# Sixteen products of 64 columns in place of three of 512 ahead of TensorE's attention loop

## The chip, the cores and the metric

The kernel runs on one core of a Trainium2 chip. The metric is the device time of one execution in microseconds (us), given as a median of several executions.

## The reference

Local attention feeds a mixture of experts, which feeds a second block with a SoLU layer. Cut to its core:

```python
def reference(**kwargs):
    # attention: batch 4, heads 8, 768 rows, head width 64; chunks of 32 rows,
    # each sees 16 rows to its left, 8 to its right and 8 memory rows
    for c in range(nc):
        k_full = np.concatenate([mem_k, k[:, :, l_start:r_end]], axis=2)
        v_full = np.concatenate([mem_v, v[:, :, l_start:r_end]], axis=2)
        scores = scale * np.matmul(q_c, k_full.transpose(0, 1, 3, 2))
        a = np.exp(scores - np.max(scores, axis=-1, keepdims=True))
        a = a / (np.sum(a, axis=-1, keepdims=True) + 1e-09)
        out[:, :, c_start:c_end] = np.matmul(a, v_full)
    x = out.transpose(0, 2, 1, 3).reshape(3072, 512)
    # experts: each token goes to one of 8, at most 384 tokens each, best logits first
    logits = x @ w_gate
    for e in range(8):
        h = np.maximum(x[assigned == e] @ w1[e], 0.0)
        y[assigned == e] = h @ w2[e]
    h = y @ w_in                      # 512 -> 1024
    solu = h * softmax(h)
    ln = (solu - mean) / sqrt(var + 1e-06) * g_ln
    return ln @ w_out
```

## The kernel before, in words

The program is written engine by engine: each engine has its own block of code, and the order in it is the order of execution. Semaphores alone join the engines. There is no scheduler.

The attention works on NT = 24 tiles of 128 token rows. For each tile, SyncE loads one packed tile of q and k (`unit`, 768 KB, four buffers) and one of v (`vr`, 520 KB, four buffers). TensorE's code for it is the function `step` (called at L510 in a loop `pe.Fori(0, NT // DEEP)` of six passes, four steps in each pass). A step holds, in this order, pieces of different tiles, as a pipeline written out by hand:

- `x_T` (L478): four transposes of an earlier tile's attention output, for the gate;
- `values` (L467): 32 products of probabilities with v, each on 64 rows and 32 columns of the array;
- `scores` (L443): 32 products of q with k, of the same shape of array piece;
- `probs_T` (L453): four transposes of the probabilities;
- `gate` (L486): four products with the gate's weights, of eight columns each.

The loop is real: its four steps stand once in the program and run six times. Three more, shortened steps stand behind it. ScalarE copies the transposes out of PSUM and takes the exponential; VectorE finds the row maxima (L955), subtracts them (L959) and normalises (L966 to L974); GpSimd copies the result (L1386). Because the loop has no special first pass, VectorE first fills with zeros what the first steps read before it exists (L934 to L942). The very first of these memsets (L934) fills half of `pr`, the probabilities, and counts up `probs`.

SyncE's queue issues the loads in a fixed order: q and k of tile 0, the two small inputs `wg` (L409) and `gain` (L410), then the tiles. From tile 2 of v and tile 4 of q and k on, a load waits until the products of an earlier tile are through. The stores to `x_rows` stand behind all loads in that queue.

Ahead of its loop TensorE waits for the first memset, multiplies that zero half of `pr` with itself WARM times into the PSUM bank `PT_PS` (L505), which nothing reads before it is written again, and then waits for the constants and for both small inputs (`small_in` at 32):

```python
pe.wait_ge(probs, 1)
blank = pr[:, 1, :, :, :].rearrange("p h a w -> p (h a w)")
for _ in range(WARM):
    nc.tensor.matmul(PT_PS[:, :], blank[:, 0:P], blank, start=True, stop=True)
pe.wait_ge(consts, 1)
pe.wait_ge(small_in, 32)
with pe.Fori(0, NT // DEEP) as b:
    for r in range(DEEP):
        step(b * DEEP + r, r, b + 1)
```

Behind the attention come a search for the experts' thresholds (VectorE, with small products at L532 and L536) and eight experts, each of some hundreds of large products (L563 to L565 and others), written out in full. A product of float32 operands is carried out as two weight loads and two products; a transpose of float32 as one of each.

Of the kernel before, what the change touches and what calls it, by code (L numbers as in the profile page):

```python
# [32 lines left out]
P = 128  # L33
B, H, S, D = 4, 8, 768, 64
CHUNK, LEFT, RIGHT, MEM = 32, 16, 8, 8
# [15 lines left out]
KEPT = NT - DEEP  # L51
BLANK_PT, BLANK_X, BLANK_XT, BLANK_SHIFTED, BLANK_GATE = 2, 3, 4, 2, 4
TG = 12
WARM = 3
G = E * TG
NEG = -1.0e38
MARK = 1000.0
# [56 lines left out]
def build(nc, qk_in, v_in, w_gate, w1, w2, w_in, w_out, g_ln, out):  # L114
    ctx = ExitStack()
    with ctx:
# [217 lines left out]
        PT_PS, XT_PS = PS[6], PS[7]  # L334
# [97 lines left out]
        def _(pe):  # L432
# [69 lines left out]
            pe.wait_ge(probs, 1)  # L502
            blank = pr[:, 1, :, :, :].rearrange("p h a w -> p (h a w)")
            for _ in range(WARM):
                nc.tensor.matmul(PT_PS[:, :], blank[:, 0:P], blank, start=True, stop=True)  # L505
            pe.wait_ge(consts, 1)
            pe.wait_ge(small_in, 32)
            with pe.Fori(0, NT // DEEP) as b:
# [423 lines left out]
        def _(ve):  # L932
# [116 lines left out]
            def search(f, js):  # L1049
                for _, j in js:  # L1050
                    if j > 0:
                        refine(f, j - 1)
                    count(f, j)
# [209 lines left out]
            def expert(s, first=False, last=False):  # L1263
                f = s + 1
                _, rh, ro, ry = counts_for(f)
                for g in range(KF):
                    search(f, rh[g][:1])
# [263 lines left out]
```

## Time and profile before

| what | before |
|---|---|
| median of three runs | 750.47 us |
| the three runs | 747.77, 750.47, 753.61 us |
| the profiled execution's own time | 746.67 us |
| its span, first to last instruction | 745.0 us |
| mean granted TensorE clock | 0.961 |
| TensorE busy | 698.9 us (94%) |
| VectorE busy | 527.3 us (71%) |
| ScalarE busy | 328.2 us (44%) |
| GpSimd busy | 321.5 us (43%) |

PE is TensorE's products and PEld its weight loads, which overlap them; DVE is VectorE, ACT ScalarE, POOL GpSimd, SPq SyncE's queue. L505 is line 505 of the kernel. Times in the views count from the first instruction. A wait put down to "issue" is one for which the profile shows no semaphore. PEclk is the clock granted to TensorE, 1.00 for 2.4 GHz and 0.50 for 1.2 GHz. DMA queues: q1 carries SyncE's transfers and q0 GpSimd's; q8 and q14 are marked "instruction".

### The profile page before, as it was taken

To read this page: it belongs to the slowest core of one execution; us is meant where nothing else is said; L and a number is where in the kernel's file an instruction comes from. 1 tells how busy PE (TensorE), PEld (TensorE's weight loads), DVE (VectorE), ACT (ScalarE), POOL (GpSimd) and SP (SyncE) were. 2 spreads that over 40 slices of the span, in tenths; PEclk is the share of its full clock that TensorE was granted. 3 is DMA by queue.
4 is the path that set the end of the run, shared out by engine and by line. 5 is a ranking of instruction groups with operands and counts; after the bars stand their busy time and mean duration, and the time that the engine had idled before them with its cause. 6 is when DMAs were issued, how large, how long until landed. Compare 5 with 4: busy or idle time off the path is not lost.

```text
span 745.0 us, 18035 instructions
## 1 busy us (share of the span) xinstructions
PE 698.9 (94%) x7190; PEld 623.6 (84%) x7190; DVE 527.3 (71%) x1920; ACT 328.2 (44%) x537; POOL 321.5 (43%) x242
## 2 busy tenths in 40 slices
PE   7999963699999999999999999999999999999992
PEld 5899952599798889988998899889988998999881
DVE  4667658787888788778877887788778887442240
ACT  1455536341573257225722572257225713571360
POOL 2111107782673177317821772177217722762011
PEclk8999975699999999999999999999999999999997
DMA  8999993621331133013301330133013302330001
GB/s 314 350 380 389 353 370 119 195 74 38 99 106 57 57 114 107 37 57 113 114 29 57 114 114 29 56 114 113 29 63 109 113 29 71 107 106 30 0 15 42
DMA packets 24925, 89.09 MB, mean 120 GB/s; under 512 B 3360, under 2 KB 3360, under 8 KB 24864
## 3 DMA queue, kind: packets, MB, share of 16 engines
q0 software_dynamic: 13056, 46.14, 18.8%
q1 hardware_dynamic: 11808, 42.17, 15.0%
q8 instruction: 34, 0.56, 0.3%
q14 instruction: 27, 0.22, 0.1%
HBM read 75.71 MB, written 12.58 MB: 119 GB/s over the span
## 4 chain that ended last, share of the span: by engine, by line
PE 92%; DVE 5%; issue 1%; ACT 1%; POOL 0%; DVEq 0%; POOLq 0%
PE banks L563 26%; PE banks L565 24%; PE banks L564 24%; PE banks L486 3%; PE banks L592 3%; PE banks L467 3%; PE banks L443 3%; PE bank L453 2%; PE bank L478 2%; PE banks L576 1%; PE bank L556 1%; PE bank L505 1%; DVE flips L1061 1%; DVE hot_b L1073 1%; DVE xl L1260 0%
## 5 line engine op out<-in xcount | busy, mean ns | idle before, releaser
L1414 POOL TENSOR_TENSOR wl<-raw,wh 128x1024 fp32r<-128x1024 f32 x60 | 146.1, 2435 | 30.9 <-ACT wh L779 30.0
L1408 POOL DMA_INDIRECT raw<-w,w_idx x60 | 67.9, 1132 | 149.0 <-DVE w_idx L1124 111.9
L563 PE MATMUL banks<-xh,wh 128*128 128x384 f32 x256 | 90.4, 353 | 2.1 <-DVE xl L1260 2.1
L563 PE MATMUL banks<-hh,wh 128*128 128x384 f32 x256 | 90.2, 352 | 0.0
L565 PE MATMUL banks<-xh,wl 128*128 128x384 f32 x256 | 86.3, 337 | 0.0
L565 PE MATMUL banks<-hh,wl 128*128 128x384 f32 x256 | 86.2, 337 | 0.0
L564 PE MATMUL banks<-xl,wh 128*128 128x384 f32 x256 | 86.0, 336 | 0.0
L564 PE MATMUL banks<-hl,wh 128*128 128x384 f32 x256 | 85.8, 335 | 0.0
L563 PE MATMUL banks<-wout_h,uh 128*128 128x512 f32 x192 | 79.0, 411 | 0.0
L563 PE MATMUL banks<-win_h,yh 128*128 128x512 f32 x192 | 77.4, 403 | 0.0
L779 ACT ACTIVATE wh<-raw 128x1024 fp32r<-128x1024 f32 x60 | 63.4, 1056 | 28.7 <-DMA raw<-w,w_idx 28.5
L565 PE MATMUL banks<-wout_h,ul 128*128 128x512 f32 x192 | 75.4, 393 | 0.0
L564 PE MATMUL banks<-wout_l,uh 128*128 128x512 f32 x192 | 75.0, 391 | 0.0
L565 PE MATMUL banks<-win_h,yl 128*128 128x512 f32 x192 | 75.0, 391 | 0.0
L564 PE MATMUL banks<-win_l,yh 128*128 128x512 f32 x192 | 74.8, 390 | 0.0
L877 ACT ACTIVATE yh<-banks 128x384 fp32r<-128x384 f32 x32 | 15.7, 492 | 112.7 <-PE banks L565 112.7
L884 ACT ACTIVATE z<-banks 128x512 f32<-128x512 f32 x48 | 28.8, 599 | 81.9 <-PE banks L565 81.6
L1024 DVE TENSOR_SCALAR_CACHE_REDUCE hits<-VB,bank 96x256 bf16<-96x256 f32 x120 | 57.5, 479 | 4.3
L563 PEld LDWEIGHTS banks<-xh,wh 128*128 128x128 f32 x256 | 48.5, 189 | 5.4 <-issue 3.1
L563 PEld LDWEIGHTS banks<-hh,wh 128*128 128x128 f32 x256 | 48.3, 189 | 2.6
L1024 DVE TENSOR_SCALAR_CACHE_REDUCE mask<-VB,bank 96x256 bf16<-96x256 f32 x105 | 49.9, 476 | 0.0
L1024 DVE TENSOR_SCALAR_CACHE_REDUCE hot_a<-VB,bank 96x256 bf16<-96x256 f32 x105 | 49.9, 475 | 0.0
(204 smaller groups left out, 1563.7 us busy)
## 6 DMA issues: line engine op xcount, KB each, us to landing
unit<-qk_in SPq DMA_DIRECT2D x24, 768.0 KB, 6.4
vr<-v_in SPq DMA_DIRECT2D x24, 520.0 KB, 5.2
x_rows<-x_keep SPq DMA_DIRECT2D x20, 256.0 KB, 4.9
prep_first<-w_in SPq DMA_DIRECT2D x4, 512.0 KB, 5.7
x_rows<-x_sb SPq DMA_DIRECT2D x4, 256.0 KB, 4.5
prep_first<-w_out SPq DMA_DIRECT2D x2, 512.0 KB, 7.7
prep_rest<-w_out SPq DMA_DIRECT2D x2, 512.0 KB, 9.1
raw<-w,w_idx POOLq DMA_INDIRECT x60, 4.2
```

Source lines behind the costliest of these rows:

```text
L443: mm = nc.tensor.matmul(S_PS[r % 2][a][CHUNK * c:CHUNK * (c + 1), hp * WIN:(hp + 1) * WIN], q[rows, hp, CHUNK * c:CHUNK * (c + 1)], k[rows ...
L467: mm = nc.tensor.matmul(PW[CHUNK * c:CHUNK * (c + 1), a, hp * (D + 1):(hp + 1) * (D + 1)], pT[rows, r % 2, hp, CHUNK * c:CHUNK * (c + 1)], ...
L486: mm = nc.tensor.matmul(GATE_PS[r % 2], xT[:, r % 2, k, :], wg[:, k, :], start=(k == 0), stop=(k == KD - 1))
L563: nc.tensor.matmul(bank, stat_h, mov_h, start=first, stop=False)
L564: nc.tensor.matmul(bank, stat_h, mov_l, start=False, stop=False)
L565: return nc.tensor.matmul(bank, stat_l, mov_h, start=False, stop=last)
L592: mm = nc.tensor.transpose(TR[n % 3][:, k * P:(k + 1) * P], z[:, i, kk * P:(kk + 1) * P], ident[:, :])
L779: nc.scalar.activation(wh[:, c % WCH, :], stage(s, c), ACT.Copy).then_inc(w_hi, 1)
L884: nc.scalar.activation(z[:, g // 2, 512 * (g % 2):512 * (g % 2) + 512], MM[z_bank(s, g)][:, :], ACT.Copy)\
L1024: ins = nc.vector.tensor_scalar(hits_of[n], VB[:, :], cand[:, n:n + 1].bitcast(F32), None, ALU.is_ge, ALU.add, accum_out=cnt[:, n:n + 1])
L1408: gp.indirect_dma_start(stage(s, c), None, table, bass.IndirectOffsetOnAxis(ap=w_idx[:, c % WCH:c % WCH + 1], axis=0))\
L1414: gp.tensor_tensor(wl[:, c % WCH, :], stage(s, c), wh[:, c % WCH, :].bitcast(F32), ALU.subtract)\
```

## The change

WARM is 16 instead of 3, and each product reads 32 columns of `blank` as its weights and 64 columns as its moving operand, instead of 128 and 512. It writes 32 partitions and 64 columns of the same bank.

```diff
-WARM = 3
+WARM = 16
...
             for _ in range(WARM):
-                nc.tensor.matmul(PT_PS[:, :], blank[:, 0:P], blank, start=True, stop=True)
+                nc.tensor.matmul(PT_PS[0:CHUNK, 0:D], blank[:, 0:CHUNK], blank[:, 0:D], start=True, stop=True)
```

TensorE's order ahead of the loop, as the difference of the two programs; L505 are the zero products, L508 the loop's head:

```order
 L431 UNCONDITIONAL_BRANCH
-L505 MATMUL bank<-pr 128x512 x3
+L505 MATMUL bank<-pr 32x64 x16
 L508 UNCONDITIONAL_BRANCH
 L508 ISA
```

Nothing else differs on any engine. In TensorE's program all that stands from L508 on is thirteen source products further back than it was.

The loop's fourth step and its end, which are the same in both programs (of before; in brackets what an instruction waits for):

```order
L478 MATMUL bank<-ident,x_sb 128x128 [waits xT_sb,x_ready]
L478 MATMUL bank<-ident,x_sb 128x128 x3
L467 MATMUL banks<-vr,pT 32x65 [waits x_ready,pT_sb,v_loaded1]
L467 MATMUL banks<-vr,pT 32x65 x31
L443 MATMUL banks<-unit 32x64 [waits gate_sb,qk_loaded3,shifted]
L443 MATMUL banks<-unit 32x64 x31
L453 MATMUL bank<-ident,pr 128x128 [waits pT_sb,probs]
L453 MATMUL bank<-ident,pr 128x128 x3
L484 REGISTER_ALU
L486 MATMUL banks<-wg,xT 128x8 [waits xT_sb]
L486 MATMUL banks<-wg,xT 128x8 x3
L508 REGISTER_ALU
```

Behind them stands only the loop's COMPARE_AND_BRANCH (L508). No row of the loop moved against another; all of it stands thirteen products further back.

## Rows read from the trace of the kernel before

**Rows 1.** The page: TensorE's totals, and the chain that ended last

```profile
PE 698.9 (94%) x7190; PEld 623.6 (84%) x7190; DVE 527.3 (71%) x1920; ACT 328.2 (44%) x537; POOL 321.5 (43%) x242
...
PE 92%; DVE 5%; issue 1%; ACT 1%; POOL 0%; DVEq 0%; POOLq 0%
```

**Rows 2.** Busy time by stretch (us; instructions in brackets)

```profile
core 0: us, PE busy (x) PEld busy (x) DVE busy (x) ACT busy (x) POOL busy (x), PEclk, DMA share, GB/s
11.96:14.28 2.32, 0.00 (x0) 0.00 (x0) 0.00 (x0) 0.00 (x0) 0.00 (x0) 1.00 1.00 410
14.28:21.10 6.82, 6.81 (x209) 6.16 (x209) 2.06 (x5) 1.11 (x2) 0.00 (x0) 0.50 0.90 336
30.00:90.00 60.00, 60.00 (x2580) 54.47 (x2578) 42.08 (x95) 33.41 (x71) 10.46 (x17) 1.00 0.98 372
```

**Rows 3.** Timeline, 0 to 30 us: start, us, engine, line, operation, idle before it

```profile
1.62 5.49 PE L505 MATMUL bank<-pr 128*128 128x512 f32 x6 [1.62 <-DVE pr L934]
...
2.64 0.33 PEld L505 LDWEIGHTS bank<-pr 128*128 128x128 f32 x1 [0.52 <-issue]
...
3.49 0.33 PEld L505 LDWEIGHTS bank<-pr 128*128 128x128 f32 x1 [0.52 <-issue]
...
6.90 0.86 PE L478 MATMUL bank<-ident,x_sb 128*128 128x128 f32 x4
...
14.53 1.17 PE L443 MATMUL banks<-unit 64*32 64x64 f32 x64
...
16.54 1.71 PE L486 MATMUL banks<-wg,xT 128*128 128x8 f32 x8
...
19.13 1.19 PE L467 MATMUL banks<-vr,pT 64*32 64x65 f32 x64
...
20.17 1.11 PE L443 MATMUL banks<-unit 64*32 64x64 f32 x64
```

**Rows 4.** Where L467 breaks off: timelines at 11, 23, 98 us; chain at 99 us

```profile
11.11 0.68 PEld L467 LDWEIGHTS banks<-vr,pT 64*32 64x32 f32 x63 [0.17 <-issue]
...
14.29 0.12 PEld L467 LDWEIGHTS banks<-vr,pT 64*32 64x32 f32 x1 [2.50 <-issue]
...
23.09 0.27 PEld L467 LDWEIGHTS banks<-vr,pT 64*32 64x32 f32 x24 [0.17 <-issue]
23.57 0.50 PEld L467 LDWEIGHTS banks<-vr,pT 64*32 64x32 f32 x40 [0.21 <-issue]
...
98.39 0.58 PEld L467 LDWEIGHTS banks<-vr,pT 64*32 64x32 f32 x50 [0.17 <-issue]
...
99.12 0.91 issue
```

**Rows 5.** DMA queues: windows 11.8:12.0, 15.6:15.9, 21:21.3, 26.4:26.8, 26.8:97.5 (q14), 97.5:98

```profile
q8 instruction: 1, 0.02, 31.3%
q8 instruction: 1, 0.02, 19.7%
q8 instruction: 1, 0.02, 18.2%
q8 instruction: 1, 0.02, 13.7%
...
q14 instruction: 2, 0.02, 0.1%
...
q8 instruction: 1, 0.02, 11.7%
```

**Rows 6.** The page: instruction queue over the whole span (packets, MB, share)

```profile
q8 instruction: 34, 0.56, 0.3%
```

**Rows 7.** The second small input: its issue (timeline), then its time to landing (DMA view)

```profile
1.71 0.42 SPq L410 DMA_DIRECT2D gain<-g_ln  x1
...
gain<-g_ln SPq DMA_DIRECT2D x1, 4.0 KB, 3.8
```

**Rows 8.** Timeline of PE in the fourth step

```profile
24.14 0.85 PE L443 MATMUL banks<-unit 64*32 64x64 f32 x64
```

## The prediction

> **What bounds the kernel now.** I read the page's busy shares and chain first: TensorE (PE) holds 92% of the chain that ended last, and it is busy for 698.9 of 745.0 us [rows 1]. So what delays PE in the attention loop delays the end, unless PE waits afterwards for something else. The cut by stretches then shows where PE does not work early on [rows 2]: its products run from 1.6 us, it does nothing from 11.96 to 14.28 us, then it works at a granted clock of 0.50 (the lower level, 1.2 GHz) until 21.10 us, and from 30 to 90 us it is busy for all 60 us at 1.00 (2.4 GHz) with 2580 products, 23.3 ns each. The timeline of the opening [rows 3] shows what the change touches: six products of L505 (three in the source, each carried out as two) from 1.62 us on, 0.85 us apart by their weight loads, then the loop's first transposes of L478 at 6.90 us. The rest of the group gives what each part of a step takes at the lower clock.
>
> What stops PE at 11.96 us is no semaphore. The values products of the loop's second step (L467) break off after 63 of 64 pairs of weight load and product, and the last one starts at 14.29 us behind "issue" [rows 4]. Two more places look alike: L467 of the fourth step breaks off after 24 weight loads (0.21 us), and L467 of the second step behind the loop after 50 (in the chain 0.91 us of issue from 99.12, so the next is at 100.03 us) [rows 4]. Beside each of them stands one packet of the instruction queue q8 [rows 5]: one starts between 11.8 and 12.0 us and PE goes on at 14.29; one between 21.0 and 21.3 and PE goes on at 23.57; one between 97.5 and 98.0 and PE goes on at 100.03. So each time PE goes on some 2.4 us after its packet's start (from the middle of each window: 2.39, 2.42, 2.3). I read them as PE waiting for its code.
>
> The places fit blocks of fixed length. One step is 144 pairs, thus 288 instructions, and the waits, the ALU instruction and the like between them (rows of the order in the section on the change) make about 7 more. From pair 63 of the second step to pair 24 of the fourth there are 2 x 288 - 78 = 498, with 14 others 512. From there to load 50 behind the loop I count 116 pairs to the end of the loop, 80 of the step behind it, 4 transposes and 50 pairs: 250 pairs, 500 instructions, with some 12 others 512 again. A packet is 0.56 MB / 34 = 16.5 KB [rows 6]. Four packets start before 27 us, and none in the 70 us in which the loop repeats [rows 5]; twice 512 instructions, with one packet between the stalls whose boundary leaves no wait, means 256 instructions in a block. And each packet goes out about one block ahead of need: the one at 15.6 us comes soon after PE enters a block at 14.29, long before that block's 256 instructions are through at about 19.9 (L443 of the third step comes shortly after, at 20.17 [rows 3]). Counting on from the stall in the fourth step, the next boundary lies 256 instructions later. The loop ends after 232 instructions and some 6 others, so that boundary is about 18 instructions behind the loop's end: the loop needs blocks 0 to 4, and block 5, whose packet starts only between 26.4 and 26.8 us, is not wanted until the exit at 95 us.
>
> The Trainium skill ("Runtime: NRT & Kernel Launch", section "Instruction fetch mechanics") says that code comes in 16 KiB blocks of 256 instructions, that TensorE's buffer holds 2048 instructions, and that crossing a boundary is "mostly hidden". The trace agrees on the block and not on the cost: 2.33 us here [rows 2, 4]. By the page's "hidden" the change would come out as rival 1 below.
>
> **The change, part by part.** (a) Removed: six products, 6 x 0.85 = 5.1 us, 5.5 with the first one's start [rows 3]. (b) Added: sixteen products, each carried out as two, with 64 columns in place of 512. By columns one takes 0.85 / 8 = 0.107 us, and 32 make 3.4 us. From above, a small product behind a 128-column weight load at the lower clock takes 1.71 / 8 = 0.214 us (L486) [rows 3], and 32 make 6.8 us. The new loads have 32 columns, so I take 3.4 us: the products end near 5.1 us. (c) The loop does not start at 5.1 us: it waits for both small inputs, and the second, issued at 1.71 us, lands 3.8 us later, at 5.5 us [rows 7]. With the waits behind it I estimate 5.9 us for the first transposes instead of 6.90, 1.0 us earlier. At the lower clock a step takes 5.64 us (L443 of the second step at 14.53 to L443 of the third at 20.17 [rows 3]) and the second step up to the break another 1.6, so PE is at the break by 13.1 us, before 14.29. So (a) to (c) are worth nothing by themselves: the code wait covers them. Should the products take 6.8 us, the transposes would come at about 8.5 and PE would be at the break by 13 us at full clock (144 x 23.3 ns = 3.4 a step) and by 15.7 at the lower one: 0 or 1.4 us lost.
>
> (d) What the change moves is the code. Before, L505 is 3 x 4 = 12 instructions; now 16 x 4 = 64. All that follows lies 52 instructions further on, and each block boundary falls 52 instructions (26 pairs) earlier in the program.
> - First stall: PE breaks off after pair 37 instead of 63. Does the block still come at 14.3 us? The data transfers fill the engines then (DMA share 1.00) [rows 2], and the packet can go when what was queued before it is through; I take 14.3, with 1.2 us earlier as the other end, if it follows its request at a fixed distance. Then 26 pairs more remain: 26 x 1.11/64 (L443, the same array piece, at the lower clock [rows 3]) = +0.5 us.
> - Boundary into block 5: it moves from 18 behind the loop's end to 34 before it, near pair 61 of the scores products (L443) of the fourth step. PE gets there at 25.0 us (24.14 us + 61/64 of 0.85 [rows 8], and the 0.21 us stall becomes its own delay). The packet starts at 26.4 to 26.8 us and the code is there 2.4 us later, at 29.0. So a new wait of 4.0 us, which contains the +0.5. Lower end: the distance from the entry into a block to the next packet was 15.6 - 14.29 = 1.3 to 1.6 us at the first stall [rows 4, 5], against 2.9 at the one at 23.57; with 1.4 the code is there at 23.5 + 1.4 + 2.4 = 27.3, a wait of 2.3. Queued behind this wait are the end of the scores, with it VectorE's maximum and the next load of q and k; nothing of this is late for another reason, so the wait counts in full.
> - Clock: behind the idle 2.32 us the clock was 0.50 for 6.82 us [rows 2]. 209 products ran in it; at 23.3 ns they take 4.87 us. Loss 1.95 us. The new wait is longer than the old, so I expect the same again, +1.95 (0 to 1.95).
> - Exit: block 6 is asked for when block 5 is first entered, 70 us before it is wanted, so the 0.91 us at 99.12 us goes: -0.9. What is late next there is VectorE's normalisation, which waits for these same products, so the gain is passed on. Block 7 is then asked for near 98.7 us; it is wanted in the routing search, where PE waits for VectorE anyway.
>
> Sum: 4.0 + 1.95 - 0.9 = +5.0 us. The profiled execution took 746.67 us (its span 745.0 and 1.67 around it), so 751.7 by its measure; the median of the three runs is 750.47, and I place the forecast on it: 755.5 us. Ends: 2.3 + 0 - 0.9 = +1.4 and 4.0 + 1.95 = +6.0.
>
> **The rivals.**
> 1. No new wait: boundary hidden, or the code before the loop is padded so that the loop does not shift. Then only +0.5 - 0.9 remain, or nothing: 750.0 to 750.5 us, not slower. For it: from 14.29 to 23.5 us one boundary passes unseen. Against it: three of the five boundaries in the loop's first pass and behind the loop left one. 25%.
> 2. The new wait comes, the clock stays at 1.00 behind it: 750.5 + 4.0 - 0.9 = 753.6 us. 13%.
> 3. Not slower but faster: the block of the first stall comes 1.2 us sooner, because it is asked for sooner, the clock survives, and no new wait comes: -1.2 - 1.95 + 0.5 - 0.9, some 747 us. Against it: a shorter start leaves PE idle longer before the block. 5%.
> 4. The loop, now on six blocks with the seventh fetched ahead, no longer fits the buffer, and every pass fetches its code again. Each block then costs at least the 2.9 + 2.4 = 5.3 us from entry to use, six blocks 32 us a pass against 4 x 144 x 23.3 ns = 13.4 [rows 2]; five repeats make +93 us, 843 us. It decides as soon as the seventh block pushes out the first. For it: the trace of before never shows more than six blocks held. 5%. The skill's page named above has both rules that bear on it: 2048 instructions (eight blocks) speak against; that a taken branch leaves a "2-page window" and must fetch speaks for, and the trace has no packet in 70 us of branching [rows 5].
>
> **How the numbers follow.** Forecast 52%, rivals 25, 13, 5 and 5. The three runs spread from 747.77 to 753.61, so a median may be off by 2 or 3 us. The range 748.5 to 759.0 holds the forecast with that spread, rivals 1 and 2, and leaves out rivals 3 and 4. One per cent is 7.5 us, about what a measurement tells from no change. Slower by over that: rival 4 and the upper tail of the forecast (the threshold is 758.0), 16%. Faster by over 1% needs under 743: 3%. Within: 81%.
>
> **What would show it.** L505: 32 products ending near 5.1 us; L478 starting at 5.9. The first break in L467 of the second step after about 37 pairs, PE on again near 14.3. A break of 2 to 4 us near pair 61 of L443 in the fourth step, with a q8 packet 2.4 us before its end, and the clock at 0.50 behind it. A q8 packet near 30 us (block 6). No issue wait in L467 at 98 us. If L443 of the fourth step runs through, my block count or the request rule is wrong; if packets recur in each pass, rival 4 holds. If the small products end after 7 us, (b) was mis-sized.

## The result, and the profile after

| | before | after |
|---|---|---|
| median | 748.36 us (20 runs) | 752.29 us (20 runs) |
| lowest and highest | 746.00, 753.83 us | 749.51, 753.35 us |
| profiled execution | 746.67 us | 753.06 us |
| its span | 745.0 us | 751.3 us |

The ratio after/before is 1.0045, 95% interval 1.0031 to 1.0059: the change made the kernel slower by 0.45%, 3.9 us between the medians. The two profiled executions lie 6.4 us apart. That of before came from the fast end of its runs and that of after from the slow end, so the traces show the mechanism but overstate its price. A second profile of the changed kernel (after_again, below) has a span of 750.2 us.

The page of the changed kernel, its lines on the span, on TensorE and its granted clock in forty slices, and on the chain:

```profile
span 751.3 us, 18087 instructions
...
PE 702.0 (93%) x7216; PEld 629.3 (84%) x7216; DVE 528.4 (70%) x1920; ACT 328.8 (44%) x537; POOL 321.3 (43%) x242
...
PEclk8599995599999999999999999999999999999997
...
PE 92%; DVE 5%; issue 1%; ACT 1%; POOL 0%; DVEq 0%; POOLq 0%
```

The shares of the chain are those of before [rows 1]; in the clock's row the second slice (18.8 to 37.6 us) has 5, where the page of before has 9. The fives further on are the routing search, which runs at the lower level in both. The cut by stretches, with the columns of [rows 2]:

```profile
1.60:6.14 4.54, 3.42 (x32) 3.27 (x33) 3.86 (x7) 0.55 (x1) 3.58 (x24) 1.00 0.93 251
10.80:13.32 2.52, 0.00 (x0) 0.00 (x0) 0.00 (x0) 0.00 (x0) 0.00 (x0) 1.00 1.00 404
14.94:38.84 23.90, 22.05 (x574) 19.60 (x572) 8.81 (x20) 6.75 (x13) 1.84 (x3) 0.50 0.72 257
```

The small products fill 3.42 of 4.54 us. PE then idles 2.5 us before its code, as before, and the low clock, which was granted for 6.82 us in [rows 2], stays from 14.94 to 38.84 us. The timeline of weight loads shows where PE breaks off, and answers to [rows 3] and [rows 4]:

```profile
1.61 3.26 PEld L505 LDWEIGHTS bank<-pr 128*32 128x32 f32 x32 [1.61 <-DVE pr L934]
...
6.14 0.42 PEld L478 LDWEIGHTS bank<-ident,x_sb 128*128 128x128 f32 x4 [1.26 <-DVE x_sb L940]
...
10.14 0.46 PEld L467 LDWEIGHTS banks<-vr,pT 64*32 64x32 f32 x37 [0.17 <-issue]
13.32 0.28 PEld L467 LDWEIGHTS banks<-vr,pT 64*32 64x32 f32 x27 [2.71 <-issue]
...
21.93 0.69 PEld L478 LDWEIGHTS bank<-ident,x_sb 128*128 128x128 f32 x3
23.74 0.18 PEld L478 LDWEIGHTS bank<-ident,x_sb 128*128 128x128 f32 x1 [1.11 <-issue]
24.14 0.95 PEld L467 LDWEIGHTS banks<-vr,pT 64*32 64x32 f32 x64 [0.22 <-issue]
25.11 0.93 PEld L443 LDWEIGHTS banks<-unit 64*32 64x32 f32 x61
27.41 0.18 PEld L443 LDWEIGHTS banks<-unit 64*32 64x32 f32 x3 [1.38 <-issue]
```

What to see: 32 weight loads of L505 (sixteen products, two each), then L467 after 37 loads (13.32 is the second step), L478 of the fourth step after three of four, and L443 of the fourth step after 61 of 64. Three breaks in the loop's first pass, each put down to "issue" and each at the instruction where the count of 256 to a block puts it. The packets of the instruction queue in windows of 0.3 us at 11.0, 21.2 and 25.0 us and of 0.4 us at 48.2 us answer to [rows 5]:

```profile
q8 instruction: 1, 0.02, 20.6%
...
q8 instruction: 1, 0.02, 18.3%
...
q8 instruction: 1, 0.02, 18.2%
...
q8 instruction: 1, 0.02, 14.6%
```

PE goes on 2.2 to 2.4 us behind each of the first three (11.15 to 13.32, 21.35 to 23.74 and 25.15 to 27.41, from the middle of each window). The fourth, for the seventh block, comes only in a later pass. The chain around the new break, of after and then of before; the last row of each is the transposes that open the seventh step:

```profile
26.28 1.14 issue
...
30.39 0.95 PE bank L478 x4
...
35.98 0.95 PE bank L478 x4
...
40.36 0.49 PE bank L478 x4
```

```profile
26.37 0.49 PE bank L478 x4
...
33.24 0.49 PE bank L478 x4
```

At 26.37 us before and at 30.39 us after, the fifth step's transposes begin: 4.0 us of the loss is there at the end of the loop's first pass. At the seventh step (33.24 against 40.36 us) it is 7.1: two more steps at the lower clock. At the exit from the loop the chain of after has no wait for code in L467, where [rows 4] has 0.91 us:

```profile
105.07 0.49 PE bank L478 x4
105.56 0.81 PE banks L467 x53
106.37 0.02 issue
...
106.83 0.70 DVE x_sb L974
```

The last normalisation starts at 106.83 us, against 100.91 before: 5.9 us of loss are left, 1.2 less than in the seventh step. From there to the end it stays between 5.9 and 6.6 us.

### The profile page after: what moved, and what is told of

Same layout as the page of the kernel before. It is cut to its first block, busy times and chain, and to the rows that moved or that the text cites. A ratio compares the mean times of both kernels' runs of the same rounds, so it can differ in the third digit from the quotient of the medians.

```text
span 751.3 us, 18087 instructions
## 1 busy us (share of the span) xinstructions
PE 702.0 (93%) x7216; PEld 629.3 (84%) x7216; DVE 528.4 (70%) x1920; ACT 328.8 (44%) x537; POOL 321.3 (43%) x242
## 4 chain that ended last, share of the span: by engine, by line
PE 92%; DVE 5%; issue 1%; ACT 1%; POOL 0%; DVEq 0%; POOLq 0%
PE banks L563 26%; PE banks L565 24%; PE banks L564 24%; PE banks L486 3%; PE banks L467 3%; PE banks L592 3%; PE banks L443 3%; PE bank L453 2%; PE bank L478 2%; PE banks L576 1%; DVE flips L1061 1%; PE bank L556 1%; DVE hot_b L1073 1%; DVE xl L1260 0%; DVE hot_b L1164 0%
## 5 line engine op out<-in xcount | busy, mean ns | idle before, releaser
L563 PEld LDWEIGHTS banks<-xh,wh 128*128 128x128 f32 x256 | 48.6, 190 | 5.4 <-issue 3.1
```

The costliest lines, as they stand in the source:

```text
L563: nc.tensor.matmul(bank, stat_h, mov_h, start=first, stop=False)
```

## The experiments

The code-position theory is that of the prediction: what counts is where the code stands, since PE waits for new blocks of 256 instructions in the loop's first pass. The main rival is that the sixteen products do too little work for the clock. "More instructions" is against before. Each ratio is to executions of before on the same chip.

| kernel | more instructions | ratio to before | 95% interval |
|---|---|---|---|
| no product (none0) | -12 | 1.0007 | 0.9982 to 1.0033 |
| 3 small (small3) | 0 | 1.0029 | 1.0002 to 1.0057 |
| 16 small in a loop (loop16) | about 6 | 1.0003 | 0.9980 to 1.0025 |
| 7 small (small7) | 16 | 0.9992 | 0.9969 to 1.0014 |
| 8 small (small8) | 20 | 1.0024 | 1.0006 to 1.0041 |
| 16 small again (after_again) | 52 | 1.0056 | 1.0037 to 1.0076 |
| 3 large and 13 small (big3_small13) | 52 | 1.0064 | 1.0045 to 1.0082 |
| 16 small, loads held (hold_after) | 52 | 1.0053 | 1.0033 to 1.0074 |
| 48 tiny (pad48) | 180 | 1.0060 | 1.0032 to 1.0087 |
| before, loads held (hold_before) | 0 | 1.0011 | 0.9986 to 1.0035 |
| before, shorter look-ahead (look3_before) | 0 | 0.9998 | 0.9976 to 1.0020 |

**Work taken away, code left in place.**

```diff
 # small3, against the changed kernel
-WARM = 16
+WARM = 3
```

> Three small products in place of the three large ones: the same 12 instructions, so the code stands where it stood before; only the work ahead of the loop is less (0.64 us by after's 0.107 us each). Code-position theory: L467 of the second step breaks off after pair 63, L443 of the fourth step runs through, the issue wait of about 0.9 us at the loop's exit is there; time as before, ratio 0.999 to 1.001. Rival (the missing warm-up work costs the time, because the clock is low when the loop begins): slower by at least the change's 0.45%, ratio 1.0045 or more.

L467 of the second step broke after 63 loads, as in before, and L443 of the fourth ran through; the wait at the exit was there, but of 0.36 us, not 0.9. The time is undecided: 1.0029 excludes neither a small loss nor almost none, and its twelve runs spread from 745.5 to 755.9 us. Taking the products away altogether was the sharper question.

```diff
 # none0
-WARM = 16
+WARM = 0
```

> No products ahead of the loop at all: 12 instructions fewer than before, so block 5 begins at 1230, well behind the loop, and L467 of the second step breaks in the scores products' first pairs or just ahead of them (instruction 462 of my numbering: after about five pairs of L443). Code-position theory: the missing work is covered by the code wait, ratio 0.999 to 1.002. Rival (missing work leaves the clock low in the first steps and the clock then costs): ratio 1.003 or more, as the three small products' 1.0029 with its wide interval allows.

1.0007 with no work at all ahead of the loop speaks against the rival, though the interval (up to 1.0033) just reaches the 1.003 that it asked for; loop16 below decides. A row with the columns of [rows 2], then the chain, show why so little is lost:

```profile
5.80:14.65 8.85, 8.73 (x276) 7.87 (x276) 3.05 (x6) 0.63 (x1) 0.00 (x0) 1.00 0.97 384
```

```profile
5.92 1.09 PE bank L478 x4
...
17.35 1.54 issue
...
22.27 1.64 issue
...
26.50 0.49 PE bank L478 x4
```

The loop begins at 5.92 us at the pace of the lower level: four transposes take 1.09 us where after took 0.63, and until 14.65 us a product takes 8.73 / 276 = 31.6 ns (6.81 / 209 = 32.6 at a granted 0.50 and 23.3 at 1.00 in [rows 2]). The row's PEclk says 1.00 all the same, so that column cannot be relied on in this opening. PE is so slow that the block for which before waited 2.33 us is there almost when PE needs it; then it waits 1.54 us for the next block and 1.64 us for the one after. At 26.50 us the fifth step's transposes start: in before it was 26.37. Fast or slow at the start, PE did not get through the first pass sooner than its code.

**Work kept, code moved.**

```diff
 # big3_small13, against before
             for _ in range(WARM):
                 nc.tensor.matmul(PT_PS[:, :], blank[:, 0:P], blank, start=True, stop=True)
+            for _ in range(13):
+                nc.tensor.matmul(PT_PS[0:CHUNK, 0:D], blank[:, 0:CHUNK], blank[:, 0:D], start=True, stop=True)
```

> The three large products stay and thirteen small ones follow them: 64 instructions as in the changed kernel, and more work ahead of the loop than in either (5.5 + 1.4 us). Code-position theory: breaks after pair 37 of L467 in the second step and after pair 61 of L443 in the fourth, no issue wait at the exit, ratio near the change's, 1.003 to 1.006 (up to 0.001 more for the 1.4 us, if the code wait does not cover them). Rival (missing work): ratio 1.000 to 1.002.

More work ahead of the loop than in any other kernel, and as slow as the change. The issue waits in its chain, up to 28 us:

```profile
13.51 1.23 issue
...
18.07 0.31 issue
...
21.62 2.68 issue
...
26.78 1.49 issue
```

They stand where those of after stand, and one more (0.31 us) at the boundary after 18 pairs of L467 in the third step. In this run the clock was at 1.00 until 24.4 us, so PE came to its boundaries early and waited 5.7 us in all; after, slower, waited 4.4 (2.55, 0.71 and 1.14). In these two traces the clock of the first pass and its waits trade against each other.

**The same sixteen products, short code.**

```diff
 # loop16, against the changed kernel
-            for _ in range(WARM):
-                nc.tensor.matmul(PT_PS[0:CHUNK, 0:D], blank[:, 0:CHUNK], blank[:, 0:D], start=True, stop=True)
+            with pe.Fori(0, WARM // 4):
+                for _ in range(4):
+                    nc.tensor.matmul(PT_PS[0:CHUNK, 0:D], blank[:, 0:CHUNK], blank[:, 0:D], start=True, stop=True)
```

> The same sixteen small products as in the changed kernel, written as a loop of four passes with four products each: 16 instructions and some 7 for the loop, about 11 more than before instead of 52. Code-position theory: block 5 begins behind the attention loop again; L467 of the second step breaks near pair 57, no wait for code at the end of the first pass, exit wait present; ratio 0.999 to 1.002, clearly below the changed kernel's in this batch. Rival (these sixteen products do too little for TensorE's clock): ratio as the changed kernel's, 1.0045.

> The changed kernel itself once more, as the measure for the other two on this chip. Both theories: ratio 1.003 to 1.006; breaks after pair 37 of L467 and pair 61 of L443, exit without wait.

This is the plainest pair: 1.0003 against 1.0056 on one chip, the intervals apart, with the same sixteen products executed. The weight loads of loop16:

```profile
11.45 0.66 PEld L467 LDWEIGHTS banks<-vr,pT 64*32 64x32 f32 x60 [0.17 <-issue]
13.90 0.18 PEld L467 LDWEIGHTS banks<-vr,pT 64*32 64x32 f32 x4 [1.78 <-issue]
...
24.47 0.95 PEld L467 LDWEIGHTS banks<-vr,pT 64*32 64x32 f32 x64 [0.33 <-issue]
```

The break comes after 60 loads, so the loop costs 6 instructions more than before's three products, not the 11 I had guessed. L467 of the fourth step (24.47) is whole and so is what follows it, and the wait at the exit is there (0.39 us in its chain). The changed kernel's loss comes from writing its sixteen products out, 46 instructions more than this loop, and not from what they compute.

**The edge: seven against eight products.**

```diff
-WARM = 16
+WARM = 7     # small7
+WARM = 8     # small8
```

> Seven small products, 28 instructions: 16 more than before. By my count block 5 then begins at instruction 1202 of my numbering and the loop's branch is 1200, so the loop still needs five blocks. Code-position theory: L467 of the second step breaks after pair 55, no wait of 1 us or more at the end of the loop's first pass, the exit wait stays; ratio 0.999 to 1.002. Rival (missing work): between three and sixteen small products, ratio 1.004 or more.

> Eight small products, 32 instructions: only four more than with seven, but block 5 begins at 1198, inside the loop by its last two or three instructions. Code-position theory: a wait for code of 1 to 4 us at the end of the first pass (behind the gate products of the fourth step, before the transposes of the next), no issue wait at the exit, and a ratio above that of seven small products by 0.002 to 0.005. Rival (missing work): no difference from seven beyond 0.001.

The weight loads of small7, then of small8:

```profile
11.33 0.61 PEld L467 LDWEIGHTS banks<-vr,pT 64*32 64x32 f32 x55 [0.17 <-issue]
14.57 0.16 PEld L467 LDWEIGHTS banks<-vr,pT 64*32 64x32 f32 x9 [2.63 <-issue]
...
27.57 0.51 PEld L478 LDWEIGHTS bank<-ident,x_sb 128*128 128x128 f32 x4
```

```profile
12.60 0.85 PEld L467 LDWEIGHTS banks<-vr,pT 64*32 64x32 f32 x53 [0.33 <-issue]
13.79 0.21 PEld L467 LDWEIGHTS banks<-vr,pT 64*32 64x32 f32 x11 [0.33 <-issue]
...
17.03 0.38 PEld L467 LDWEIGHTS banks<-vr,pT 64*32 64x32 f32 x34 [0.17 <-issue]
18.43 0.42 PEld L467 LDWEIGHTS banks<-vr,pT 64*32 64x32 f32 x30 [1.03 <-issue]
...
28.25 0.42 PEld L478 LDWEIGHTS bank<-ident,x_sb 128*128 128x128 f32 x4 [1.37 <-issue]
```

In small7 the fourth step is followed at once by the fifth (27.57 us has no wait ahead of it). In small8, four instructions later, the transposes that open the fifth step wait 1.37 us for code, at 28.25 us: the boundary is at the loop's branch, where the count has it. The breaks in L467 (55 and 53 loads) agree too. At the exit small7 has a wait of 0.43 us in L467, small8 none. The ratios differ by 0.0032, as expected, though their intervals overlap from 1.0006 to 1.0014: the trace is clear here, the time alone would not be.

**The count with another remainder.**

```diff
 # pad48, against the changed kernel
-WARM = 16
+WARM = 48
-                nc.tensor.matmul(PT_PS[0:CHUNK, 0:D], blank[:, 0:CHUNK], blank[:, 0:D], start=True, stop=True)
+                nc.tensor.matmul(PT_PS[0:CHUNK, 0:8], blank[:, 0:CHUNK], blank[:, 0:8], start=True, stop=True)
```

> Forty-eight tiny products (8 columns each): 192 instructions, 180 more than before. By the count the blocks now begin at 14 (just ahead of the loop), 270, 526, 782, 1038 and 1294 of my numbering; the loop (17 to 1200) has four boundaries inside. Breaks: L443 of the first step after pair 55 or 56, L443 of the second after pair 36, L443 of the third after pair 16 or 17, L467 of the fourth after pair 62; none near the loop's end; no issue wait in L467 at the exit. Each boundary costs up to the 3.7 to 5.4 us from one entry to the next block's arrival, less the 2 to 3 us of work in a block. Code-position theory: one boundary more than before in the first pass, ratio 1.001 to 1.005. Rival (only a boundary in the loop's tail hurts): ratio 0.998 to 1.000, with the exit wait of 0.9 us saved.

```profile
8.83 0.88 PEld L443 LDWEIGHTS banks<-unit 64*32 64x32 f32 x56
13.16 0.20 PEld L443 LDWEIGHTS banks<-unit 64*32 64x32 f32 x8 [3.45 <-issue]
...
24.87 0.68 PEld L467 LDWEIGHTS banks<-vr,pT 64*32 64x32 f32 x62 [0.17 <-issue]
28.82 0.14 PEld L467 LDWEIGHTS banks<-vr,pT 64*32 64x32 f32 x2 [3.26 <-issue]
```

L443 of the first step breaks after 56 loads and L467 of the fourth after 62, both as counted; the two boundaries between left no wait of their own in this run, and the chain has no wait for code at the exit. The rival that only a boundary in the loop's tail costs falls: here the tail is free of one, and 1.0060 is as slow as the change. What all the runs fit is the number of blocks that still have to be fetched while PE goes through the first pass: four here and in after, three in before. In the chains of the thirteen traces the transposes that open the fifth step start between 26.2 and 28.7 us in the seven kernels with three such blocks, at 28.3 us in small8 and between 29.9 and 32.2 us in the five others with four. Small8, whose fourth block begins only at the loop's branch, lost less by its ratio too (1.0024); whether the place of the block makes that difference is not shown, since its interval overlaps that of after_again.

**Less data ahead of the packets.**

```diff
 # hold_before and hold_after: q and k of tile 2
                 if u >= DEEP:
                     sp.wait_ge(scores_ps, u - DEEP + 1)
+                elif u == 2:
+                    sp.wait_ge(pv_ps, 1)
 # look3_before: in place of both
+                if u >= 3:
+                    sp.wait_ge(scores_ps, u - 2)
+                elif u == 2:
+                    sp.wait_ge(pv_ps, 1)
```

> The kernel of before, but SyncE issues q and k of tile 2 only once the first values products are through (about 8.6 us) instead of at 3.6 us. The code stands where it stood. Theory (a code packet goes behind the data that was queued before it): 0.79 MB less is queued, at 0.38 MB/us about 2 us, so the first packet starts near 9.5 to 10 us instead of 11.9, the break after pair 63 shrinks from 2.3 us to under 1 us, and the ratio to before is 0.994 to 0.999. Rival (a packet has a fixed delay behind its request, about 3 us): the packet starts at 11.5 to 12 us as before, ratio 0.999 to 1.001. Second rival: q and k of tile 2 come late and the third step waits for them, ratio above 1.001.

> The changed kernel with the same hold on tile 2's q and k. Queue theory: the break after pair 37 of L467 shrinks by 1.5 us or more; those of the fourth step (after three transposes, after pair 61 of L443) stay, since the block positions are the change's; ratio to before 1.000 to 1.003, below the change's 1.0045. Fixed-delay rival: ratio 1.003 to 1.006.

> The kernel of before with the hold, and with every load of q and k from tile 3 on issued one step later (three tiles ahead, not four), so that less data is queued ahead of every packet. Queue theory: the later packets of the first pass also start sooner after their requests (1 to 1.5 us instead of 1.4 to 3), the waits of 0.2 us in the fourth step and 0.9 us at the exit shrink; ratio 0.993 to 0.999. Rival: three tiles ahead is too little for a landing time of 6 us and a step of 3.4 us, PE waits for q and k, ratio above 1.002.

The weight loads of hold_before:

```profile
10.19 0.68 PEld L469 LDWEIGHTS banks<-vr,pT 64*32 64x32 f32 x63 [0.17 <-issue]
12.71 0.12 PEld L469 LDWEIGHTS banks<-vr,pT 64*32 64x32 f32 x1 [1.83 <-issue]
...
23.13 0.42 PEld L469 LDWEIGHTS banks<-vr,pT 64*32 64x32 f32 x24 [0.33 <-issue]
24.27 0.67 PEld L469 LDWEIGHTS banks<-vr,pT 64*32 64x32 f32 x40 [0.72 <-issue]
```

The first block came 1.6 us sooner (12.71 against 14.29 us), its packet 1.5 us (in a window of 0.3 us from 10.3 us on, against 11.9). Most of that is not the held data: PE itself was 0.9 us further on in this execution (the scores products of the first step load from 7.51 us, in before from 8.44), partly because its zero products ended at 6.41 us, in before at 7.11, so it also entered the block before sooner. Some 0.6 us is left for the 0.79 MB, where I expected 2, and PE's wait shrank from 2.33 to 1.67 us, not to under 1. Hold_after against after gives the same: block 0.78 us sooner (12.54 against 13.32), PE 0.23 us further on (7.24 against 7.47), 0.55 left; its first break shrank from 2.7 to 2.2 us, not by 1.5, and its ratio is the change's. So neither of the two theories, the queue and the fixed delay, holds in full.

Nothing was won by it. In hold_before the wait in the fourth step grew from 0.21 to 0.72 us, and the clock fell earlier and stayed low longer (12.40 to 32.88 us); this profile is the slowest of that kernel's twelve runs (753.36 us, median 750.00). That the held data then stood in the queue ahead of the later packets may be the reason for the longer wait, but is not shown.

With the shorter look-ahead the wait in the fourth step was gone, but the third step had one of 0.94 us by its loads, and the one at the exit did not shrink, as expected, but grew from 0.91 to 2.01 us:

```profile
98.89 2.01 issue
```

The fifth step began at 26.18 us in its chain, against 26.37 in before, which no measured time shows. None of the eleven kernels is faster than before beyond its interval.

## Why the prediction was right or wrong

The median of 752.29 us lies in the range, and the direction (slower) and the place of the new wait were right: +5.0 us (0.67%) was forecast and +3.9 us (0.45%) measured. Two steps failed.

The first is the step from the sum to the chances. With three runs of before in hand I took one per cent as "about what a measurement tells from no change", and so put 81% on "within 1%" although my own sum said slower by 0.67%. Literally 0.45% is within 1%, but the interval of the measurement is 0.14% to either side, and a loss of 0.45% stands clear of it: the change made the kernel slower, and the chances should have said what the sum said.

The second is the largest term of the sum, the new wait of 4.0 us. It measured 1.14 us in the profile of after and 1.80 us in the second one. That the sum still came near the result is in part luck: the clock took what the wait did not.

Point by point:

- **(a) to (c), the products themselves.** Right in size: 32 loads in 3.3 us, an end at 5.0 us, and L478 at 6.17 us (5.9 forecast). Right that the code wait covers it, as far as none0 tells: without any work ahead of the loop the ratio is 1.0007, though its interval leaves room for 0.3%. The 6.90 us that I took from before as the start of the transposes belongs to one execution: behind the same six products they started at 6.24 us in hold_before and at 5.99 in look3_before.
- **(d) the code moves.** Right to the pair: 37 in the second step, 61 in the fourth.
- **First stall.** The block came at 13.32 us, 1.0 us earlier than I took, near the other end that I had named (1.2 us, a packet at a fixed distance behind its request). PE was 0.97 us further on there (the first step's scores products load from 7.47 us, in before from 8.44) and the boundary 26 pairs or 0.3 us earlier in the code, so it entered the block before some 1.3 us sooner.
- **The boundary before the fourth step's L467.** Missed. I let the 0.21 us of before vanish, but the block was late again, and PE waited 0.71 us (1.38 in the second profile, 2.68 in big3_small13's chain). Its packet started 3.4 us or more behind the entry into the block before it (near 17.8 us, after some 18 pairs of the third step's L467, where big3_small13 breaks; the packet between 21.2 and 21.5 us), where before had 1.3 us.
- **The new wait of 4.0 us, the term that failed.** I had PE there at 25.0 us at full clock and the block at 29.0. PE came at 26.28 us, since the clock was low from 14.94 us on, and the block at 27.41 us, since its packet followed the entry into the block before it by some 1.4 us (23.74 to 25.15), which was my lower end, and not by 2.9. The sum at that place was nevertheless 4.0 us, because the low clock had taken what the wait did not.
- **Clock, +1.95 us.** Too small in this execution: between the fifth step and the seventh the loss grew by 3.1 us, since the lower level held until 38.84 us. I priced it as one spell behind one wait; there were three waits, and the two later ones (0.71 and 1.14 us) came before the clock had risen again. The clock differs from run to run (the second profile of after has it low until 35.5 us, with 3.4 us at full level in between), so no price of a single profile is that of the median. How much of the 3.9 us is wait and how much is clock is open: I found no kernel that keeps the one and drops the other.
- **Exit, -0.9 us.** Right, and 1.2 us by the normalisations' starts.
- **Base.** I added the sum to the median of three runs, 750.47 us; twenty gave 748.36. Of the 3.2 us by which 755.5 was too high, 2.1 are this.
- **Rival 1** (no new wait) is refuted by the trace of after. **Rival 2** needed the clock to stay, and it did not. **Rival 3**: its first part came, the block 1.0 us sooner, but the clock fell and the new wait was there. **Rival 4**: the seventh block was fetched, and no packet followed it until the exit, so at least seven blocks are held. The Trainium skill ("Runtime: NRT & Kernel Launch", "Instruction fetch mechanics") gives 2048 instructions for TensorE, which these runs fit, though none shows more than seven blocks (1792) held. Its rule that a taken branch whose target lies outside the current window of two pages must fetch it again they contradict: between 48.6 and 107 us of after the loop went on branching back over its six blocks, and q8 sent no packet.
- **My rule for when a packet is asked for** (on entry into the block before) failed for the seventh block (number 6): due near 30 us, its packet came near 48 us, near 61 in the second profile and near 72 in small8. It cost nothing, and what triggers it stays open.

Small3's 1.0029 also stays open. It has before's code, and less work; no work at all gave 1.0007. I take it for scatter of the clock, but that is not shown.

## What to carry to other kernels

In this kernel unrolled instructions ahead of a hardware loop were not free, even though an idle engine executed them, because they moved the loop against the blocks in which code is fetched. Where the trace shows an engine breaking off in the middle of a group behind "issue", count instructions between such breaks and look for packets of the instruction queue ahead of each. A warm-up or a filler may be better written as a short loop of its own: sixteen products in four passes cost nothing measurable here (1.0003, interval 0.9980 to 1.0025), and the same sixteen written out cost 0.5%.

## What was unexpected of the hardware

- A packet of 16.5 KB, sent while the data queue kept the DMA engines full, let TensorE go on 2.2 to 2.4 us after its start in before and after (up to 3.0 us in none0: packet between 20.8 and 21.0 us, PE on at 23.91). It started 1.3 to 3.7 us after PE had entered the block before it, by the count of instructions. So a block took some 3.7 to 6 us to arrive in these two traces, while PE executes its 128 pairs in 3.0 us at full clock (23.3 ns each [rows 2]): in the first pass code sets the pace. With some 32 ns a product for its first 8.7 us and no zero products ahead of the loop, none0 ended that pass within 0.13 us of before.
- The clock fell at the end of PE's first wait for code in before (14.28 us), 1.6 us after it in after (14.94) and within it in the second profile of after (near 11.6, PE on at 13.20). The lower level lasted 6.8 us in one profile of before and 23.9 us in one of after, where short waits for code kept falling between stretches of work.
- Taking 0.79 MB off the queue, about 2 us of transfer, moved the next code packet by only some 0.6 us, once PE's own head start of 0.9 us is taken off the 1.5 us that the trace shows, and no time was won.
